# Blank products on TensorE ahead of and between the first scores, another order in the first period, and a last gate in three parts, in a fused attention and feed-forward kernel

## The reference, cut to what matters

```python
# attention: q, k, v of (4, 8, 576, 64); rotary embedding on q and k
def rotate(x):
    x1, x2 = (x[..., :half], x[..., half:])
    return np.concatenate([x1 * cos - x2 * sin, x1 * sin + x2 * cos], axis=-1)
scores = scale * np.matmul(rotate(q), rotate(k).transpose(0, 1, 3, 2))
attn = exp(scores - max(scores)); attn = attn / (sum(attn) + 1e-09)
x = (attn @ v), heads side by side        # (2304, 512)
# feed-forward: w_in (512, 2048), w_out (2048, 512), alpha (2048)
h = x @ w_in
g = np.maximum(h, 0.0) + alpha * np.minimum(h, 0.0)
out = g @ w_out                            # (2304, 512)
```

## Time and profile before

| what | value |
|---|---|
| time, median of 3 runs | 699.22 us (698.68 to 699.78) |
| the profiled execution's own time | 698.69 us |
| its span in the profile | 696.9 us |
| PE busy | 676.4 us (97%) |
| DVE, ACT, POOL busy | 368.8, 316.2, 281.5 us (53%, 45%, 40%) |
| mean DMA rate | 74 GB/s |

### The profile page before, as it was taken

How to read it: one execution, slowest core, us unless ns; L and a number is a source line. 1 busy time by engine, 2 the same in 40 slices (tenths; PEclk the granted TensorE clock), 3 DMA queues, 4 the chain that set the end, 5 groups by cost and what they waited for, 6 DMA issues and landing times.

```text
span 696.9 us, 12112 instructions
## 1 busy us (share of the span) xinstructions
PE 676.4 (97%) x4100; PEld 588.3 (84%) x4100; DVE 368.8 (53%) x677; ACT 316.2 (45%) x744; POOL 281.5 (40%) x258
## 2 busy tenths in 40 slices
PE   3899999999999999999999999999999999999996
PEld 2788888888888887698889999999999999999995
DVE  4688888888888887545542343233323323432231
ACT  2677777777777776433333223222222232223222
POOL 5656677777776503222222222222222222222221
PEclk9999999999999999999999999999999999999999
DMA  6898555666666643600001000000000010001001
GB/s 153 218 226 211 138 135 135 141 143 143 143 143 139 150 113 89 240 1 1 0 2 46 0 1 16 32 0 1 30 15 0 0 45 0 0 0 46 1 1 46
DMA packets 76619, 51.30 MB, mean 74 GB/s; under 512 B 61088, under 2 KB 61472, under 8 KB 76064
## 3 DMA queue, kind: packets, MB, share of 16 engines
q1 hardware_dynamic: 76576, 50.76, 29.0%
HBM read 22.95 MB, written 4.72 MB: 40 GB/s over the span
## 4 chain that ended last, share of the span: by engine, by line
PE 76%; issue 16%; POOL 2%; DVE 2%; DMA 1%; SPq 0%; ACT 0%; POOLq 0%; DVEq 0%; ACTq 0%
PE banks L629 19%; PE banks L656 19%; PE banks L553 14%; PE banks L511 12%; PE banks L575 10%; POOL g_lo L455 2%; PE banks L571 2%; DVE pt L916 0%; DMA k_two<-k_hi 0%; DMA raw_q<-in_q 0%; DVE nmax L867 0%; DMA out<-stage 0%; DVE k_lo L892 0%; DVE prob L1035 0%; ACT stage L828 0%
## 5 line engine op out<-in xcount | busy, mean ns | idle before, releaser
L455 POOL TENSOR_TENSOR g_lo<-g,g_hi 128x384 fp32r<-128x384 f32 x96 | 99.4, 1035 | 308.8 <-ACT g_hi L816 299.6
L981 DVE TENSOR_SCALAR g<-banks,alpha_sb 128x384 f32<-128x384 f32 x96 | 59.3, 618 | 250.9 <-ACT pos L808 250.9
L629 PE MATMUL banks<-x_hi,w_in_lo 128*128 128x384 f32 x384 | 129.5, 337 | 0.0
L629 PE MATMUL banks<-x_hi,w_in_hi 128*128 128x384 f32 x384 | 129.5, 337 | 0.0
L629 PE MATMUL banks<-x_lo,w_in_hi 128*128 128x384 f32 x384 | 129.2, 337 | 0.0
L808 ACT ACTIVATE pos<-banks 128x384 f32<-128x384 f32 x96 | 47.2, 491 | 170.2 <-PE banks L629 170.2
L867 DVE TENSOR_REDUCE nmax<-banks 128x1 f32<-128x576 f32 x144 | 108.7, 755 | 25.7 <-PE banks L511 20.7
L656 PE MATMUL banks<-w_out_hi,g_hi 128*128 128x512 f32 x288 | 114.9, 399 | 1.6 <-POOL g_lo L455 1.4
L656 PE MATMUL banks<-w_out_hi,g_lo 128*128 128x512 f32 x288 | 113.0, 392 | 0.0
L656 PE MATMUL banks<-w_out_lo,g_hi 128*128 128x512 f32 x288 | 112.1, 389 | 0.0
L816 ACT ACTIVATE g_hi<-g 128x384 fp32r<-128x384 f32 x96 | 50.4, 525 | 115.9 <-DVE g L984 115.9
(11 more groups left out here) (85 smaller groups left out, 907.5 us busy)
## 6 DMA issues: line engine op xcount, KB each, us to landing
k_two<-k_hi SPq DMA_DIRECT2D x64, 160.0 KB, 2.9
out<-stage SPq DMA_DIRECT2D x18, 256.0 KB, 2.0
raw_q<-in_q SPq DMA_DIRECT2D x32, 128.0 KB, 2.7
raw_k<-in_k SPq DMA_DIRECT2D x32, 128.0 KB, 2.4
q_two<-q_hi SPq DMA_DIRECT2D x32, 128.0 KB, 2.3
q_two<-q_lo SPq DMA_DIRECT2D x32, 128.0 KB, 2.3
q_own<-q_hi SPq DMA_DIRECT2D x32, 128.0 KB, 2.4
raw_v<-in_v SPq DMA_DIRECT2D x32, 128.0 KB, 2.3
```

The source lines that it names most:

```text
L455: nc.gpsimd.tensor_tensor(g_lo[f % 2][:, :], g[f % 2][:, :], g_hi[f % 2][:, :].bitcast(F32), ALU.subtract).then_inc(g_lo_done, 1)
L629: mm = nc.tensor.matmul(h_ps[f % 2], w[:, j, cols], xx[:, j, :], start=(step == 0), stop=(step == 3 * CT - 1))
L981: nc.vector.tensor_scalar(g[f % 2][:, :], h_ps[f % 2], 0.0, alpha_sb[:, f:f + 1], ALU.min, ALU.mult).then_inc(neg_done, 1)
```

## The change

At the start VectorE clears a tile `blank`, and TensorE multiplies it with itself, with results that nobody reads: 16 times before the first transposes, 4 and 6 times around the transposes of k, and 3 times ahead of every tile of period 0 but the first (`run_in`). In period 0 three tiles instead of two do without the stacks, U_K and U_MIXED are turned after tile 5 instead of after tile 3, ScalarE and VectorE follow with one tile earlier, and the load of k of pair 2 is issued after the stacks of pair 1. The `sin` table and half of the first `k_two` stack are issued by ScalarE. Some early waits ask for fewer cleared tiles. At the end the last gate goes in three parts of 128 tokens through VectorE, ScalarE, GpSimd and TensorE, and there are three staging buffers.

```diff
-FIRST_TILES = (1, 2)
+FIRST_TILES = (1, 2, 3)
...
-        stage = [sb(ctx, f"stage{i}", [P, DM]) for i in range(2)]
+        stage = [sb(ctx, f"stage{i}", [P, DM]) for i in range(MT)]
...
+        def parts(i, c, f):
+
+            if is_final(i, c) and f == FT - 1:
+                return [slice(m * P, (m + 1) * P) for m in range(MT)]
+            return [slice(0, CHUNK)]
...
-            sp.dma_start(sin_sb[:, :, :], sin).then_inc(sin_in, 16)
...
-            stack(0, 0, 1)
+            sp.wait_ge(evac[U_K % T_BANKS], evac_count(-1, U_K))
+            sp.wait_ge(evac[U_MIXED % T_BANKS], evac_count(-1, U_MIXED))
+            for head, own in ((0, slice(0, D)), (1, slice(D, P))):
+                sp.dma_start(k_two[0][own, head, :].bitcast(F32), k_hi[0][own, :].bitcast(F32)).then_inc(k_two_in, 16)
...
-                    if has_pair(p + 2):
+                    if has_pair(p + 2) and not is_opening(p):
                         load(p + 2, 1)
                     if has_pair(p + 1):
                         stack(p + 1, (t + 1) % 2, 0)
                         stack(p + 1, (t + 1) % 2, 1)
+                    if is_opening(p):
+                        load(p + 2, 1)
...
-                    sp.dma_start(out[bass.ds(n * P, P), :], stage[(c * MT + m) % 2][:, :]).then_inc(
-                        stored[(c * MT + m) % 2], 16)
+                    sp.dma_start(out[bass.ds(n * P, P), :], stage[m][:, :]).then_inc(stored[m], 16)
...
+                for m, part in enumerate(parts(i, c, f)):
+                    pool.wait_ge(g_hi_done, n + 1 + m)
+                    if m == 0 and not (is_first(i, c) and f < 2):
+                        pool.wait_ge(g_used, n - 1)
+                    nc.gpsimd.tensor_tensor(g_lo[f % 2][:, part], g[f % 2][:, part], g_hi[f % 2][:, part].bitcast(F32),
+                                            ALU.subtract).then_inc(g_lo_done, 1)
...
+            def run_in(count):
+
+                for _ in range(count):
+                    nc.tensor.matmul(banks[:, 7, 0:P], blank[:, :], blank[:, :], start=True, stop=True)
+
             def score(p, t, n):
 
                 if not has_now(p):
                     return
+                if isinstance(p, int) and p == 0 and n:
+                    run_in(3)
...
-                turn(p, t, U_K)
-                turn(p, t, U_MIXED)
+                if not is_opening(p):
+                    turn(p, t, U_K)
+                    turn(p, t, U_MIXED)
...
                 for m in range(MT):
+                    if m and len(parts(i, c, f)) > 1:
+                        pe.wait_ge(g_lo_done, n + 1 + m)
...
+            pe.wait_ge(blank_done, 1)
+            run_in(16)
             pe.wait_ge(ident_in, 16)
-            for u in (*OF_NEXT, U_MIXED):
-                turn(-1, -1, u)
+            turn(-1, -1, U_Q)
+            run_in(4)
+            turn(-1, -1, U_K)
+            turn(-1, -1, U_MIXED)
+            run_in(6)
...
+                    if isinstance(p, int) and p == 0:
+                        act.wait_ge(scored, FIRST_TILES[-1] + 1)
...
-            act.wait_ge(padded, PADDED)
+            act.dma_start(sin_sb[:, :, :], sin).then_inc(sin_in, 16)
+            act.wait_ge(padded, 4)
...
+            for own, head, other in ((slice(0, D), 0, slice(D, P)), (slice(D, P), 1, slice(0, D))):
+                act.dma_start(k_two[0][other, head, :].bitcast(F32), k_hi[0][own, :].bitcast(F32)).then_inc(k_two_in, 16)
...
+                if is_opening(p):
+                    maxima(p, t, B_TILES[0])
                 lo(p, U_K, t)
                 lo(p, U_MIXED, t)
```

More of the change, by code:

```diff
@@ L50, in build @@
     PERIODS = NB * PAIRS
-    PADDED = 15
+    PADDED = 14
     W_COLS = F // (2 * PAIRS)
@@ L174, in build @@
             zero = sb(att, "zero", [P, 1])
+            blank = sb(att, "blank", [P, P])
         attention_bytes, used[0] = used[0], 0
@@ L220, in build @@
         first_step = sem("first_step")
+        blank_done = sem("blank_done")
         q_two_in, k_two_in = sem("q_two_in"), sem("k_two_in")
@@ L248, in build @@
         staged = sem("staged")
-        stored = [sem("stored0"), sem("stored1")]
+        stored = [sem(f"stored{i}") for i in range(MT)]
         block = ctx.enter_context(nc.Block())
@@ L266, in chunks, with is_opening @@
             chunk(NCHUNK // 2 - 1, 1)
+        def is_opening(p):
+            return isinstance(p, int) and p == 0
         def is_first(i, c):
@@ L361, in chunk @@
                     sp.wait_ge(staged, n + 1)
-                    sp.dma_start(out[bass.ds(n * P, P), :], stage[(c * MT + m) % 2][:, :]).then_inc(
-                        stored[(c * MT + m) % 2], 16)
+                    sp.dma_start(out[bass.ds(n * P, P), :], stage[m][:, :]).then_inc(stored[m], 16)
             chunks(sp, chunk)
             for s in stored:
-                sp.wait_ge(s, 16 * NCHUNK * MT // 2)
+                sp.wait_ge(s, 16 * NCHUNK)
         @block.gpsimd
@@ L421, in _ @@
             pool.wait_ge(padded, PADDED)
+            pool.wait_ge(blank_done, 2)
             pool.wait_ge(sin_in, 16)
@@ L775, in period @@
                 exps(p, t, A_TILES[2])
+                if is_opening(p):
+                    exps(p, t, A_TILES[3])
                 hi(p, U_K, t)
                 hi(p, U_MIXED, t)
-                exps(p, t, A_TILES[3])
+                if not is_opening(p):
+                    exps(p, t, A_TILES[3])
                 if not has_now(p):
@@ L812, in high @@
                 n = (i * 2 + c) * FT + f
[L813 to L816, removed]
+                for m, part in enumerate(parts(i, c, f)):
+                    act.wait_ge(g_done, n + 1 + m)
+                    if m == 0 and not (isinstance(n, int) and n < 2):
+                        act.wait_ge(g_used, n - 1)
+                    nc.scalar.activation(g_hi[f % 2][:, part], g[f % 2][:, part], ACT.Copy).then_inc(g_hi_done, 1)
             def to_stage(i, c, m):
@@ L824, in to_stage @@
                     act.wait_ge(g_used, (i * 2 + c + 1) * FT)
[L825 to L828, removed]
+                if not is_first(i, c):
+                    act.wait_ge(stored[m], (i * 2 + c) * 16)
+                nc.scalar.activation(stage[m][:, :], y_ps[c % 2][m], ACT.Copy).then_inc(staged, 1)
             HEADS = (slice(0, D), slice(D, P))
-            act.wait_ge(padded, PADDED)
+            act.dma_start(sin_sb[:, :, :], sin).then_inc(sin_in, 16)
+            act.wait_ge(padded, 4)
             nc.scalar.activation(prob_rem[REM:P, 0:1], raw_v[0][REM:P, QT, 0:1], ACT.Exp)
@@ L835, in _ @@
                 hi(-1, u, -1)
+            act.wait_ge(evac[U_K % T_BANKS], evac_count(-1, U_K))
+            act.wait_ge(evac[U_MIXED % T_BANKS], evac_count(-1, U_MIXED))
+            for own, head, other in ((slice(0, D), 0, slice(D, P)), (slice(D, P), 1, slice(0, D))):
+                act.dma_start(k_two[0][other, head, :].bitcast(F32), k_hi[0][own, :].bitcast(F32)).then_inc(k_two_in, 16)
             def batch(b):
@@ L980, in gate @@
                     dve.wait_ge(g_lo_done, n - 1)
[L981 to L985, removed]
+                for m, part in enumerate(parts(i, c, f)):
+                    nc.vector.tensor_scalar(g[f % 2][:, part], h_ps[f % 2][:, part], 0.0, alpha_sb[:, f:f + 1],
+                                            ALU.min, ALU.mult).then_inc(neg_done, 1)
+                    dve.wait_ge(neg_done, n + 1 + m)
+                    nc.vector.tensor_tensor(g[f % 2][:, part], g[f % 2][:, part], pos[f % 2][:, part],
+                                            ALU.add).then_inc(g_done, 1)
             def period(b, t):
@@ L1012, in period @@
                         split_x(0, 0, j)
-                maxima(p, t, B_TILES[0])
+                if not is_opening(p):
+                    maxima(p, t, B_TILES[0])
                 maxima(p, t, B_TILES[1])
@@ L1024, in period @@
                 normalise(p, *before, 1)
-            nc.vector.memset(zero[:, :], 0.0).then_inc(padded, 1)
-            dve.wait_ge(padded, PADDED)
+            nc.vector.memset(blank[:, :], 0.0).then_inc(blank_done, 1)
+            nc.vector.memset(zero[:, :], 0.0).then_inc(blank_done, 1)
+            dve.wait_ge(padded, 2)
             dve.wait_ge(sin_in, 16)
```

## The result

The changed kernel takes 696.63 us (median of 8 runs, 696.01 to 697.33) beside 698.56 us (8 runs, 698.10 to 699.78) for the kernel before, a ratio of 0.9971 with a 95% interval from 0.996 to 0.9981: 2.0 us faster. The forecast was 695.4 (for itself 694.7 to 696.0) and 3.85 us faster. Ratios count every execution and medians leave stragglers aside, so that the two can differ: of the 17 executions of the kernel before that were timed beside e1 to e4, four took 701.2 to 702.5 us at a mean granted clock of 0.993 to 0.998. The profiled execution took 696.57 us, its span is 694.7 where that of before was 696.9.

What follows compares the result with a forecast made beforehand. TensorE, 97% busy, was taken as the bound, so only opening and end could give time: 1.15 + 2.7 = 3.85 us off 699.22 gave 695.4. Its own range was 694.7 to 696.0, the wide one 694.0 to 697.3.

Steps and rivals of the forecast that it cites:

- the end: Behind the last h: gate in parts and a third staging buffer have the last tile staged 2.7 us earlier, bounds 2.3 to 2.9.
- the opening: Up to the turn of k in period 1: 1.15 us of the lead left after GpSimd's late load.
- The start: Before tile 0: moving `sin` saves 0.4 us, faster transposes of k 0.5; tile 0 at 12.6 instead of 13.54.
- Period 0: Nine tiles, 1.46 us each with three blank products, and 31 transposes: period 1 starts at 28.5 instead of 30.04.
- The blanks run in TensorE's waits: Period 0: blank products cost 0.06 us a tile, 0.5 in all, instead of 5.3 without this cover.
- The stacks: SyncE's queue for pair 1: stacks start at 20.1, the 0.91 us stall for `k_two` goes, lead 2.4.
- The moved load is late next: k of pair 2 lands at 30.1 to 30.8, so TensorE's turn in period 1 waits for GpSimd; 1.15 us of lead left.
- The clock stays low: Rival for the opening: blank products may not raise the clock, low until 24 us; 701.1 us; 5 in 100.
- The stores hold each other: Rival at the end: the third store gains only TensorE's 1.35 us; 696.7 us; 6 in 100.

Runs made afterwards that it cites:

- e1: The kernel before with the changed end alone (last gate in three parts, three staging buffers): 695.93 us, ratio 0.9947.
- e4: The changed kernel without the blank products between the tiles of period 0, those ahead of the first scores kept: 698.35 us, ratio 0.9981.
- e6: e3 with one blank product instead of three between the tiles of period 0: 694.37 us, ratio 0.9925.
- e3: The changed kernel with the load of v of pair 0 behind the stacks of pair 1, k of pair 2 loaded in its old place: 694.71 us.
- e9: The kernel before with three staging buffers and nothing else: 697.48 us, ratio 0.9993.
- e10: The kernel before with the last gate in three parts and two staging buffers: 697.57 us, ratio 0.9981.
- e2: The changed kernel with the load of k of pair 2 issued again ahead of the stacks of pair 1: 695.72 us, ratio 0.9945.
- e5: The changed kernel without any blank product, its orders, stacks and end kept: 699.93 us, ratio 1.0006.

## Why the prediction was right, and where it failed

The range held the time and the direction was right, but the gain is half of the forecast, 1.9 instead of 3.85 by the medians. The time misses the forecast's own range of 694.7 to 696.0 and is held by the wide one, which was drawn for the rivals. The nearness of 695.4 to 696.63 is in part luck: it was counted from 699.22, the median of three runs, and eight gave 698.56; from there the sum gives 694.7. In the sum's two terms, the end gave 2.5 of 2.7 and the opening nothing of 1.15.

- **The start.** Predicted tile 0 at 12.6, it was 12.89. The clock came up as assumed. The transposes of k gave the 0.5; `sin` gave 0.2 instead of 0.4, since VectorE began at 5.09 instead of 5.29. (The wait into which the six blank products had to fit was 1.77, not 2.2; they fitted, with 0.64 left.)
- **Period 0.** A step that failed, by 0.7: it took 16.6 us instead of 15.9. I gave a tile with its three blank products 1.46 us; from 14.52 to 16.37 it is 1.85: 0.99 for a tile on 64 rows instead of 0.8, and 0.86 for the blank products with the change of operands instead of 0.66. Period 1 began at 29.51 instead of 28.5. "The blanks run in TensorE's waits" was too kind: with one instead of three period 1 begins 1.9 earlier (e6). Yet with none the clock falls (e4).
- **The stacks.** The other step that failed. SyncE began the q stack of pair 1 at 21.19 instead of 20.1. `q_lo` was ready at 20.41 + 0.69 = 21.10, and SyncE's own queue ran without a pause until 20.63 + 0.52 = 21.15, so both chains were late by 1. In the queue it was `sin` (0.2), the two `k_two` issues with 1.54 instead of 1.24, and one issue of v that took 1.15 instead of 0.59: a period 0 in time would by itself not have moved the stacks. The stall for `k_two` did go.
- **The moved load is late next.** The mechanism was right and its own terms held; it inherited the lateness of the stacks: the third issue of `raw_k` at 28.83 instead of 27.7, landing 2.5 later as assumed, k turned at 36.37 instead of 35.25. Of the 1.15 that the sum had left to the turn, 0.03 remained. That the moved load is what the turn waits for is shown by e3: with its issue early and that of v behind the stacks, the turn comes at 34.85 and the time falls by 1.9.
- **The end.** Predicted 2.7, measured 2.5; e9 and e10 give the two terms as 1.3 and 1.2. TensorE began at 689.14 for a positive part at 686.98, 2.16 behind it, where I had 688.7 - 686.67 = 2.0: GpSimd's operations of 128 columns took 1.63 / 3 = 0.54 instead of 0.43.
- **The rivals.** "The clock stays low" came true where the blank products are left out, and it didn't only concern the rise: I had not thought of a fall behind a wait. *The stores hold each other* has with 696.7 nearly the measured time, but not what happened: the last staging waits for no store, and the end gives 2.5.

What is left open: e2's gain of 0.9 and the loss of the changed opening against the old one (696.63 to 695.93, e1) are inside the intervals of the ratios. The executions of e1 (695.69 to 696.02) and of the changed kernel (696.01 to 697.33) do not overlap but for 0.01, so a small loss is likely; but the two were not timed side by side, and two profiled executions with the same opening differ by 0.5 us at the last gate (686.52 in e1, 687.01 in e10). What makes the difference was not separated.

## What to carry to other kernels

Where a queue of DMA issues runs without a pause, a load moved behind others is late by their whole length; look for the one whose user comes last (here v) and move that. Filling waits with blank products pays as far as the clock would otherwise fall (none against three: 1.7 us by the medians); past that they can be work in the way, though here one instead of three gave no time that could be told apart, so the count has to be tried. A chain at the end of a kernel is worth cutting into parts and giving buffers of its own: it was 0.36% here (2.5 us), all of the gain, in a kernel whose TensorE is 97% busy.

## What was not expected of the hardware

- The granted clock falls in the middle of a run, and stays low for a while although TensorE is then fully busy: 0.50 from 39.6 to 43.0 behind waits of 2.50 (e4) and 3.06 us (e5), not behind the 1.09 of the changed kernel; and in e4 from 15.7 to 25.9, with no blank products between the scores of period 0. Four executions of the kernel before, too, took 701.2 to 702.5 at a mean clock below 1.0.
- Until past 22 us of a run the column of the granted clock can say 1.00 while the durations are those of the lower level.
- One DMA issue on SyncE's queue takes 0.5 to 0.7 us as a rule, and now and then up to 1.7, with nothing that the profile shows as a wait. In e6:

```profile
22.28 0.60 SPq L311 DMA_DIRECT2D q_two<-q_hi  x1
22.92 1.72 SPq L312 DMA_DIRECT2D q_two<-q_lo  x1
```
